# Seven row buffers instead of three in the bias part of an attention and expert kernel, and ScalarE makes the last group of features in three of four sets

## What is computed

```python
psi_rel = np.log1p(np.abs(rel))                       # rel = query position - key position
psi_i = np.log1p(np.maximum(pos[:, None], 1.0))
x = (psi_rel / psi_i)[..., None]
h = np.maximum(x @ w1 + b1, 0.0)                      # 576 x 576 x 32
bias = h @ w2                                         # 576 x 576 x 8 heads
scores = scores + bias.transpose(2, 0, 1)[None, :, :, :]
attn = softmax(scores); out = attn @ v
```

## Time and profile before

| | |
|---|---|
| median of 3 runs | 1106.88 us (1106.65 to 1109.77) |
| the profiled execution | 1105.64 us, span in the trace 1103.9 us |
| mean granted clock of PE | 0.987 |
| PE busy | 1058.7 us, 96% |
| VectorE busy | 683.1 us, 62% |
| ScalarE busy | 620.5 us, 56% |
| bytes moved | 92.18 MB, mean 84 GB/s |

### The profile page before, as it was taken

One profiled execution on the slowest core, in us unless ns is written; L12 is line 12 of the kernel. 1 busy time (PEld: TensorE's weight loads), 2 busy tenths in 40 slices (PEclk: granted clock), 3 DMA queues, 4 the chain that ended last, 5 costly groups with the idle time before them and its releaser, 6 DMA issues. The chain is left out here.

```text
span 1103.9 us, 19585 instructions
## 1 busy us (share of the span) xinstructions
PE 1058.7 (96%) x6802; PEld 837.5 (76%) x6802; DVE 683.1 (62%) x1537; ACT 620.5 (56%) x1306; POOL 91.0 (8%) x134
## 2 busy tenths in 40 slices
PE   5779999999999899999999999999999999999995
PEld 2346666666666699999999999999987888888883
DVE  6977777777778687665756656658753351632320
ACT  4767766676768676665556556556631352622320
POOL 0000000000000000000000100101012331332211
PEclk9999999999999999999999999999998999999997
DMA  6673252352432340000000000101115251531110
GB/s 180 235 250 90 50 173 54 75 152 69 103 98 83 109 161 21 29 29 9 22 30 29 29 1 29 72 7 67 54 39 188 105 211 41 192 111 39 43 38 25
DMA packets 103348, 92.18 MB, mean 84 GB/s; under 512 B 63434, under 2 KB 75082, under 8 KB 103242
## 3 DMA queue, kind: packets, MB, share of 16 engines
q1 hardware_dynamic: 98010, 79.33, 22.9%
q0 software_dynamic: 4192, 11.07, 3.0%
q10 hardware_dynamic: 1056, 0.61, 0.2%
HBM read 66.19 MB, written 25.73 MB: 83 GB/s over the span
## 5 line engine op out<-in xcount | busy, mean ns | idle before, releaser
L1005 PE MATMUL score<-dl_xt,dl_weights 128*128 128x384 f32 x1152 | 220.6, 339 | 0.0
L1005 PEld LDWEIGHTS score<-dl_xt,dl_weights 128*128 128x128 f32 x1152 | 201.8, 188 | 5.0
L586 ACT ACTIVATE at_prob<-at_neg,at_negmax 128x576 f32<-128x576 f32 (+1 forms) x160 | 124.6, 779 | 51.1 <-DVE at_negmax L664 42.0
L1169 ACT ACTIVATE dl_val<-score 128x384 f32<-128x384 f32 x96 | 47.1, 491 | 147.2 <-PE score L1005 146.5
L1259 DVE SCALAR_TENSOR_TENSOR dl_sq<-dl_sq,dl_val 128x384 f32<-128x384 f32 x96 | 53.5, 558 | 113.3 <-ACT dl_sq L1171 113.1
L664 DVE CUSTOM_DVE_ANT_0 at_neg<-score,at_bias 128x576 f32<-128x576 f32 (+1 forms) x160 | 113.9, 748 | 5.0 <-PE score L416 4.5
L1784 PE MATMUL o_acc<-dl_weights,ex_ht_hi 128*128 128x512 f32 (+1 forms) x336 | 109.7, 408 | 2.5 <-issue 2.5
L1753 PE MATMUL score<-dl_weights,ex_xt_hi 128*128 128x512 f32 x336 | 107.3, 401 | 1.4 <-DVE ex_xt_lo L1875 1.4
L431 PE MATMUL o_acc<-at_prob_t,at_v_nat 128*64 128x512 f32 (+1 forms) x320 | 85.7, 616 | 0.6 <-DVE at_o_sb L692 0.6
L1468 POOL DMA_INDIRECT slot_dram<-slot_rows,slot_i x18 | 18.1, 1007 | 772.6 <-DVE slot_i L1340 768.1
L424 PEld LDWEIGHTS pt_b<-id_sb,at_prob 128*128 128x128 f32 (+1 forms) x320 | 32.0, 140 | 62.9 <-issue 48.7
(11 more groups left out here) (217 smaller groups left out, 2164.3 us busy)
## 6 DMA issues: line engine op xcount, KB each, us to landing
dl_raw<-in_moe_w SPq DMA_DIRECT2D x12, 1024.0 KB, 5.7
bias_dram<-at_rows_sb SPq DMA_DIRECT2D x36, 288.0 KB, 2.8
ex_raw_b<-in_moe_w SPq DMA_DIRECT2D x8, 1024.0 KB, 5.9
at_bias<-bias_dram SPq DMA_DIRECT2D x3, 2304.0 KB, 9.3
at_v_nat<-in_v SPq DMA_DIRECT2D x16, 288.0 KB, 3.0
dl_x_nat<-x_dram SPq DMA_DIRECT2D x18, 256.0 KB, 3.0
x_dram<-dl_x_sb SPq DMA_DIRECT2D x6, 768.0 KB, 3.5
at_k_nat<-in_k SPq DMA_DIRECT2D x32, 128.0 KB, 2.8
```

The costliest lines, as they stand in the source:

```text
L586: nc.scalar.activation(prob[n % 2][0:m, c, :], neg[c][n % 2][0:m, :], ACT.Exp, bias=negmax[c][n % 2][0:m, 0:1], scale=-1.0, accum_out=tota ...
L1005: last = nc.tensor.matmul(h_ps[m % NHB][:, 0:CN], w[f // KT][:, k, fc], x[c % 2][:, k, :], start=k == 0 and n == 0, stop=k == KT - 1 and n ...
L1169: nc.scalar.activation(val[m % 2][:, :], h, ACT.Square).then_inc(act_step, 1)
```

## The change

Four more row buffers are formed out of the two buffers `prob`, which stand idle until the first exponential: `rows_sb` becomes a list of seven, in the order own 0, prob0 half 0, prob0 half 1, prob1 half 0, prob1 half 1, own 1, own 2. ScalarE makes group 3 in the sets with s % 4 != 3, 27 instead of 18; the count that PE waits for and the choice of `shift` follow. ScalarE makes feature 1 ahead of its first rows. Before the first exponential it waits for the last store out of each of the four halves.

```diff
--- before.py
+++ after.py
@@ -172,12 +172,12 @@
         MID = KTP // 2
         MAIN = (QT - 1) * P
         NQK, NV = 2, 3
-        NF, NR = 3, 3
+        NF, NR = 3, 7
         ACT_GROUP = 3
         TILE_SETS = P // SET
 
         feat = [buf(f"feat{i}", [P, 4, S]) for i in range(NF)]
-        rows_sb = [buf(f"rows_sb{i}", [P, S]) for i in range(NR)]
+        rows_own = [buf(f"rows_sb{i}", [P, S]) for i in range(3)]
         dist_sb = buf("dist_sb", [P, DISTW])
         bias = [buf("bias0", [P, QT, 2, S])]
         q_nat = [buf(f"q_nat{i}", [P, QT, 2 * D]) for i in range(NQK)]
@@ -187,6 +187,7 @@
         x_sb = [buf(f"x_sb{i}", [P, QT, 2 * D]) for i in range(2)]
         o_sb = buf("o_sb", [P, S])
         prob = [buf(f"prob{i}", [P, 2, S]) for i in range(2)]
+        rows_sb = [rows_own[0][:, :]] + [prob[i][:, c, :] for i in range(2) for c in range(2)] + [r[:, :] for r in rows_own[1:]]
         v_nat = [buf(f"v_nat{i}", [P, KTP, D]) for i in range(NV)]
         prob_t = [buf("prob_t0", [P, KTP, S])]
         neg = [[buf(f"neg{c}{i}", [P, S]) for i in range(2)] for c in range(2)]
@@ -240,7 +241,11 @@
 
         def by_scalar(s):
 
-            return s % 2 == 0
+            return s % 4 != 3
+
+        def by_scalar_upto(s):
+
+            return s + 1 - (s + 1) // 4
 
         def window(s, c):
             return dist_sb[:, DIST0 - (4 * s + c) * GQ:DIST0 - (4 * s + c) * GQ + S]
@@ -324,7 +329,7 @@
 
             def store_set(s):
                 sp.wait_ge(acc_read, s + 1)
-                sp.dma_start(bias_dram.rearrange("(n p) k -> n p k", p=P)[s], rows_sb[s % NR][:, :]).then_inc(rows_out[s % NR], 16)
+                sp.dma_start(bias_dram.rearrange("(n p) k -> n p k", p=P)[s], rows_sb[s % NR]).then_inc(rows_out[s % NR], 16)
 
             def load_first(t):
 
@@ -389,7 +394,7 @@
             def bias_set(s):
                 pe.wait_ge(feat_v, s + 1)
                 if by_scalar(s):
-                    pe.wait_ge(feat_a, s // 2 + 1)
+                    pe.wait_ge(feat_a, by_scalar_upto(s))
                 if s >= 2:
                     pe.wait_ge(acc_read, s - 1)
                 for half in range(2):
@@ -565,8 +570,8 @@
                 act.wait_ge(acc_ready, s + 1)
                 if s >= NR:
                     act.wait_ge(rows_out[s % NR], 16 * (s // NR))
-                nc.scalar.activation(rows_sb[s % NR][:, :].rearrange("p (a c) -> p a c", a=2), score[s % 2][:, :, 0:HALF],
-                                     ACT.Identity, bias=shift[s % 2][:, 0:1],
+                nc.scalar.activation(rows_sb[s % NR].rearrange("p (a c) -> p a c", a=2), score[s % 2][:, :, 0:HALF],
+                                     ACT.Identity, bias=shift[0 if by_scalar(s) else 1][:, 0:1],
                                      scale=rows_scale[:, s:s + 1]).then_inc(acc_read, 1)
 
             def high(g, r):
@@ -590,6 +595,7 @@
             act.wait_ge(dist_scaled, 1)
             act.wait_ge(bounds_set, 2)
             feature(0)
+            feature(1)
             act.wait_ge(shift_done, 1)
             act.wait_ge(shift_zeroed, 1)
             nc.scalar.activation(shift[1][:, :], o_acc[:, 0:1], ACT.Identity).then_inc(shift_read, 1)
@@ -597,12 +603,14 @@
             act.wait_ge(shift_read, 2)
             act.wait_ge(scale_in, 16)
             for s in range(SETS):
-                if s + 2 < SETS and by_scalar(s):
+                if s + 2 < SETS and by_scalar(s + 2):
                     feature(s + 2)
                 bias_rows(s)
                 if s - 1 in EARLY:
                     high(0, EARLY[s - 1])
             act.wait_ge(padded, 1)
+            for i in range(1, 5):
+                act.wait_ge(rows_out[i], 16 * ((SETS - 1 - i) // NR + 1))
             for g, t in STEPS:
                 n = g * QT + t
                 m = rows(t)
```

## The result

The changed kernel takes 1097.53 us (median of 8 runs, 1095.38 to 1100.91), the one before 1106.77 in the same comparison (8 runs, 1103.37 to 1110.9): ratio 0.992, 95% interval 0.9901 to 0.9939. It is faster by 9.2 us between the medians; the forecast was 7.35 us and 1099.5 us. The profiled execution of the changed kernel took 1098.72 us, 6.92 less than that of the kernel before (1105.64), and its span is 1097.0 us.

The account below looks back on a forecast made before the run. VectorE's instruction count and two holes were taken to bound the bias part: 3.87 + 3.10 + 0.38 = 7.35 us, from 1106.88 to a forecast median of 1099.5 us. Range 1097.8 to 1103.2 us.

Parts of the forecast that it names:

- What bounds the bias part: First 71 us: VectorE's instruction count and its two holes set the length; cuts there come off the end one for one.
- Term one: Bias part: VectorE makes 117 features instead of 126, nine fewer at a pitch of 0.43 us, saving 3.87 us.
- Terms two and three: Bias part: VectorE's holes before 22.94 and 49.77 vanish with more row buffers, saving 3.10 and 0.38 us.
- The cost of ScalarE's nine features: Bias part: nine more features of 772 ns on ScalarE, costed at nothing, covered by VectorE's own pace.
- The new waits: Turn to attention: first exponential waits for last stores from the probability buffers, landed by 63.3 against 64.4, costing nothing.
- the first rival: Bias part: ScalarE or PE takes part back, start tight at VectorE's sets 4 and 5; 1100.5 to 1103 us, chance 0.14.
- ScalarE as the path: Bias part: nine dearer features cost 2.3 us, only the holes' 3.48 are gained; 1105.7 us, chance 0.03.
- The stores: Bias part: store waits move to set 7 and later, holes stay, only 3.87 us come; 1103.0 us, chance 0.05.
- The clock: Bias part: PE at 1.2 GHz loses 0.75 us a set, ten sets eat the 7.35; up to 1125 us, chance 0.03.
- The rest keeps its length: After the first score matmul: the span stays as before, 1034.1 us.

Follow-up runs that it names:

- buffers_only: Against the changed kernel: seven row buffers kept, ScalarE's share back to 18 features; 1102.09 us, ratio 0.9964 to the kernel before.
- five_buffers: Against the changed kernel: five row buffers instead of seven, ScalarE still makes 27 features; 1099.61 us, ratio 0.9936 to the kernel before.
- share_only: Against the changed kernel: three row buffers instead of seven, ScalarE still makes 27 features; 1105.62 us, ratio 0.9995 to the kernel before.
- warm_turn: Changed kernel plus unused PE matmuls, 12 before the first score matmul and 20 after the first step of scores; 1107.44 us, ratio 1.0019 to before.
- again: The changed kernel once more, unchanged; 1098.5 us, ratio 0.9925 to the kernel before.
- again2: The changed kernel another time, unchanged, as reference beside other kernels; 1097.47 us, ratio 0.9934 to the kernel before.
- warm_turn_small: Changed kernel plus 4 and 8 unused PE matmuls at the turn to attention, in four column groups and two banks; 1094.69 us, ratio 0.9894 to before.

## Why the prediction was right

**What bounds the bias part.** Shown. Its length followed VectorE's instruction count and holes in the kernels with 18, 27 and 32 features on ScalarE, and stopped doing so at 36, where ScalarE's pitch took over.

**Term one, nine features for 3.87 us.** 3.86 in the bias part, from buffers_only to the changed kernel. But it holds only behind the other part: without the buffers the same nine gave 1.55 in a profile in which PE's clock, too, cost it time. The prediction summed the terms as if each stood alone, which was right for both together and said nothing of this.

**Terms two and three, 3.10 and 0.38 us.** This is the term that was mis-sized: 3.48 forecast, 4.02 measured. The prediction took the two listed holes and missed 0.35 us of unlisted short delays of VectorE and about 0.2 us of overlap that it loses at each stop.

**The cost of ScalarE's nine features, nothing.** Right. The windows give it 10.63 + 37.43 = 48.06 us busy, for which the prediction had 48.3. The cover was real but thin: five features more still shorten the bias part by 1.80 us, nine more lengthen it by 0.45.

**The new waits.** Right; the last stores out of the probability buffers had landed when the first exponential came.

**The rivals.** The tight start of the first rival did not show in the three profiles of the changed kernel, where PE was at its quick pace by 12.2 to 12.9 us. That was partly luck: in five_buffers, share_only and warm_turn it came at 14.8 to 15.4 us, and VectorE waited 0.32 to 0.54 us before set 5, the place that the prediction named. ScalarE as the path, with the dearer instruction deciding, is refuted at 27 features (the time fell by 3.86 us of bias part). At 36 ScalarE does set the pace, though it costs 0.45 us of bias part and not 0.26 us a feature. What the Trainium skill's page "ScalarE: Activation LUTs", section "Rules for kernel authors", says of relu on VectorE holds here per instruction (771 against 524 ns), and for the sum only once ScalarE has no slack. The stores did not bind. The clock did fall, at another place and by less than the rival had it: 2.1 us at the turn, not ten sets of the bias part.

**The rest keeps its length.** Wrong in detail, nearly right in the sum: attention took 2.12 us more and the dense layer 1.61 less in the profiled execution, and behind the first score matmul stand 1034.9 us against the 1034.1 forecast. In the medians the gain was 8.0 in two comparisons beside the kernel before and 9.2 in the first, against 7.35 forecast. Of what is above the forecast 0.5 us is in the bias part; the rest is not traced to a place, and it is smaller than what single executions of one kernel differ by. The forecast of 1099.5 is a little high for that reason, and all three medians of the changed kernel, 1097.53, 1097.47 and 1098.5, lie at the low end of its range or just under it.

## What to carry to other kernels

When the engine that sets the pace is held by waits of another engine, moving work off it first fills those waits: remove what holds it, and then move the work, and count the two together. A second engine takes work for nothing only up to its own pitch per round; put both pitches side by side, as means over a round (here, from the prediction's pitches, ScalarE 1.23 against VectorE 1.40 us a set at three in four, 1.32 against 1.34 at seven in eight, 1.40 against 1.29 at all), and stop one step before they cross. Short waits of PE at a change of stages can be followed by a stretch at 1.2 GHz, here of 1.0 to 2.1 us of cost behind 2.64 us of waits; a few matmuls that nothing reads, laid in parallel column groups inside the wait, are a cheap trial. Read the start times of single instructions too: delays under 0.2 us are in no list of waits, and made up 0.35 us here.

## What was not expected of the hardware

- The clock of PE fell to 1.2 GHz for 3.4 or 6.8 us at the turn to attention in some profiles, with its start 2.0 to 4.0 us after the first score matmul, around waits of 1.04 and 1.60 us, and not in others of the same kernel (again against again2). Each 3.4 us of it made attention 1.0 us longer.
- A 128x32 by 288 column product took 0.25 us per instruction when all went to one column group and one bank (24 in 5.98 us), and 0.074 in four column groups (16 in 1.18).
- The fillers brought 2.8 to 3.8 us in the medians of three kernels, more than the 1.0 to 2.1 us of attention that a drop at the turn costs. In three of the four kernels with fillers the last stretch, from the start of the last matmul of the experts' first product on, was 27.2 to 27.5 us long, against 28.4 to 30.3 in all other profiles. The granted clock goes with it: a drop that starts 9.5 to 11.2 us into that stretch lasts 3.4 us in these three and in share_only (28.4 us, no fillers), and 6.8 us in the other ten (28.7 to 30.3). Here again2 and warm_turn_small, from where that drop starts:

```profile
1077.10:1083.90 6.80, 4.93 (x13) 3.79 (x12) 0.00 (x0) 0.00 (x0) 0.30 (x2) 0.50 0.03 10
...
1077.30:1080.70 3.40, 3.40 (x10) 2.62 (x9) 0.00 (x0) 0.00 (x0) 0.30 (x2) 0.51 0.01 4
1080.70:1087.60 6.90, 3.13 (x14) 2.20 (x12) 0.00 (x0) 0.69 (x1) 1.00 (x1) 0.99 0.03 11
```

  Why fillers 1000 us earlier should go with a shorter drop there is open; it was not tried.
